# Attention in front of two feed-forward layers: another order of work on the engines, v requested after its first sum, guards stored as columns

## Chip, cores and metric

One core of one Trainium2 chip. The metric is the device time of one execution in microseconds (us), for one core. Engines: TensorE (PE, with PEld its weight loads), VectorE (DVE), ScalarE (ACT), GpSimd (POOL), and SyncE (SP), which issues the DMAs.

## What is computed

```python
# q, k, v: (4, 8, 576, 64) float32
q_d, k_d, v_d = (t.reshape(B, H, 144, 4, D).mean(axis=3) for t in (q, k, v))
out_d = softmax_guarded(q_d @ k_d.T / 8) @ v_d          # denominator + 1e-9
out_up = np.repeat(out_d, 4, axis=2)
scores = np.where(abs(i - j) < 4, q @ k.T / 8, -1e9)    # a band of 7 keys a query
out_local = softmax_guarded(scores) @ v
x = (out_up + out_local) -> (2304, 512)
x = ((h := x @ w_in1) * sigmoid(h)) @ w_out1            # 512 -> 2048 -> 512
x = ((h := x @ w_in2) * sigmoid(1.702 * h)) @ w_out2
```

## The kernel before

Attention runs in 16 units; a unit is two heads of one batch entry, its features on 128 partitions. After it come six token blocks of the feed-forward layers (class `Ffn`), whose weights and inputs are split in a rounded part and a rest, so that each product is three TensorE matmuls. `Ffn` isn't touched by the change; its order is written out too.

In attention each engine has a program of its own, ordered by semaphores. `iterations` (L787) gives unit 0, a hardware loop up to EARLY - 1, then units written out up to 15, and a last call that only finishes unit 15. Each call of `body(u)` starts unit u and finishes unit u-1 ("old"):

- TensorE (L1165): `band_scores(u)` (L1086) writes the mask into two PSUM banks with two bfloat16 matmuls (L1091), then adds 18 matmuls of q by a window of 70 keys, one for each head h and tile t (L1098); head h uses the array's rows 64h to 64h+63 and writes output partitions 64h to 64h+63. `avg_scores(u)` (L1114, L1119) gives the scores of the averaged attention by three matmuls whose stationary operand `qavg` is block diagonal. `group(old, j)` transposes exponentials: j = 0 to 2 three band tiles each, j = 3, 4 half of the averaged ones (L1084). `band_product` (L1149) and `avg_product` (L1160) follow. Groups 3 and 4 stand between the products.
- VectorE (L1013): maxima of the band scores (L1022), subtraction (L1025), maxima of the averaged scores (L1029), `sums(u+1)`, which adds fours of q and k (L1010), row sums of the band exponentials (L1034), + 1e-9 (L1036), reciprocal (L1040), the averaged sums + 1e-9 (L1044), reciprocal (L1046), `early` (work for the first feed-forward block: L245, L256, L284), and the unit's output `x` (L1056).
- ScalarE (L950): copies of the transposed groups out of PSUM (L935, L939), the band exponential (L959), the averaged exponentials with their row sums (L972), `diagonal(u+1)` (L948), which copies q's sums into `qavg`, `oavg` (L981), and roundings for the first block.
- GpSimd (L883): normalises band and averaged exponentials (L889, L893), adds four rows of v in two steps (`vpair` L898, `vavg` L902), then two sums of first-layer weights (`sum_weights`, L905, into `G`: L912/L914 in odd units, L917/L918 in even ones).
- SyncE (L822), its requests in one queue: `load_qk(u+2)` once `band_scores(u)` and `sums(u)` are done; `load_vwin(u+1)` (v's windows); `load_vn(u+1)` once `vavg(u)` is done (`v_sum`); in odd units `first_raw` (raw weights, L113).

Before all that GpSimd makes two identities and the mask (12 small fills, L874), and TensorE runs 11 warm-up matmuls (L1184).

Of the kernel before, what the change touches and what calls it, by code (L numbers as in the profile page):

```python
# [22 lines left out]
P = 128  # L23
# [661 lines left out]
def build(nc, qkT, v, vw, w_in, w_out, out, heads):  # L685
# [7 lines left out]
    EARLY = 5  # L693
# [10 lines left out]
    AQ = 96  # L704
    NA = 2 * SD // AQ
# [10 lines left out]
    with ExitStack() as whole:  # L716
# [9 lines left out]
        with ExitStack() as ctx:  # L726
# [17 lines left out]
            qavg = sb("qavg", [P, 2, SD])  # L744
            sums4 = sb("sums4", [P, 2, SD])
            pband = [sb(f"pband{i}", [P, NT, WIN]) for i in range(2)]
            pavg = [sb(f"pavg{i}", [AQ, NA, SD]) for i in range(2)]
            mxb, smb, rcb = (sb(n, [P, NT]) for n in ("mxb", "smb", "rcb"))
            mxa, nga, sma, rca = (sb(n, [AQ, NA]) for n in ("mxa", "nga", "sma", "rca"))
            ptb = ffn.spare(NT * P).rearrange("p (t n) -> p t n", t=NT)  # L750
            pta = sb("pta", [P, 2, 2 * SD])
# [19 lines left out]
        q_diag = sem("q_diag")  # L771
        band_sc = sem("band_sc")
        avg_sc = sem("avg_sc")
        b_max, b_sub, b_exp, b_sum, b_grd, b_rcp, b_nrm = (
            sem("b_" + n) for n in ("max", "sub", "exp", "sum", "grd", "rcp", "nrm"))
# [24 lines left out]
        def _(eng):  # L800
# [13 lines left out]
            def start(u):  # L814
                load_qk(u)
                load_qk(u.after())
                load_vn(u)
                eng.wait_ge(pads, 2)
                load_vwin(u)
                load_vwin(u.after())  # L820

            def body(u, first=False):  # L822
                if not isinstance(u.n, int) or u.n + 2 < UNITS:


                    if first:
                        eng.wait_ge(avg_sc, u.n + 1)
                    else:
                        eng.wait_ge(band_sc, 2 * (u.n + 1))
                        eng.wait_ge(qk_sum, u.n + 1)  # L830
                    load_qk(u.after().after())
                if not isinstance(u.n, int) or u.n + 1 < UNITS:
# [3 lines left out]
                    eng.wait_ge(v_sum, u.n + 1)  # L836
                    load_vn(u.after())
# [19 lines left out]
        def _(eng):  # L857

            eng.memset(ident[:], 0.0).then_inc(consts_fill, 1)
            eng.memset(band[:], 0.0).then_inc(consts_fill, 1)  # L860
            eng.memset(ident16[:], 0.0).then_inc(consts_fill, 1)
            eng.wait_ge(consts_fill, 3)
            for tile in (ident, ident16):
                eng.affine_select(out=tile[:], in_=tile[:], compare_op=ALU.not_equal, fill=1.0, base=0,
                                  pattern=[[-1, P]], channel_multiplier=1).then_inc(consts, 1)
            eng.wait_ge(consts, 2)
            fills = 3
            for a in (0, 1, NT - 1):
                off = starts[a] - QT * a
                for sign in (1, -1):  # L870

                    for h in range(2):
                        part = band[h * QT:(h + 1) * QT, a, :]
                        eng.affine_select(out=part, in_=part, compare_op=ALU.is_ge, fill=NEG,  # L874
                                          base=sign * off + FACTOR - 1,
                                          pattern=[[sign, WIN]],
                                          channel_multiplier=-sign).then_inc(consts_fill, 1)
                        fills += 1

                        eng.wait_ge(consts_fill, fills)  # L880
            eng.sem_inc(consts, 1)

            def body(u, first, last):  # L883
# [5 lines left out]
                eng.tensor_tensor(e[:], e[:], rcb[:].unsqueeze(2).broadcast_to([P, NT, WIN]),  # L889
# [3 lines left out]
                eng.tensor_tensor(e[:], e[:], rca[:].unsqueeze(2).broadcast_to([AQ, NA, SD]),  # L893
                                  ALU.mult).then_inc(a_nrm, 1)
# [29 lines left out]
            eng.wait_ge(pads, 3)  # L924
# [4 lines left out]
        def _(eng):  # L929
            def group(u, j):  # L930
# [7 lines left out]
                else:  # L938
                    eng.activation(pta[0:HP, j - NLG, :], pt[bank][0:HP, 0:2 * SD],  # L939
                                   ACT.Copy).then_inc(p_cp, 1)  # L940

            def diagonal(u):

                eng.wait_ge(qk_sum, u.n + 1)
                eng.wait_ge(avg_sc, u.n)
                for h in range(2):
                    rows = slice(h * D, (h + 1) * D)
                    eng.activation(qavg[rows, h, :], sums4[rows, 0, :], ACT.Copy).then_inc(q_diag, 1)  # L948

            def body(u, first, last):  # L950
# [6 lines left out]
                if last is not None:  # L957
                    eng.wait_ge(b_sub, 2 * (u.n + 1))
                    eng.activation(pband[u.odd][:], pband[u.odd][:], ACT.Exp,  # L959
                                   scale=scale_band).then_inc(b_exp, 1)  # L960
                if not first:
                    for j in range(NLG, NG):
                        group(old, j)
                if last is not None:

                    eng.wait_ge(a_max, u.n + 1)
                    eng.activation(nga[:], mxa[:], ACT.Copy, scale=-scale_avg).then_inc(a_neg, 1)
# [3 lines left out]
                    for c in range(NA):  # L971
                        eng.activation(pavg[u.odd][:, c, :], sa[0:AQ, c * SD:(c + 1) * SD], ACT.Exp,  # L972
                                       scale=scale_avg, bias=nga[:, c:c + 1],
                                       accum_out=sma[:, c:c + 1]).then_inc(a_exp, 1)
                    if not last:
                        diagonal(u.after())

# [5 lines left out]
                if not first and isinstance(u.n, int):  # L983
                    if u.n in (5, 7, 8):
                        ffn.round_weights(eng, (5, 7, 8).index(u.n))
                    elif u.n == 6:
                        eng.wait_ge(x_done, 1 + 2)
                        ffn.round_x(eng, 0, B11)
                    elif 9 <= u.n < 15:
                        eng.wait_ge(x_done, 1 + 8)  # L990
                        ffn.round_x(eng, 0, FILLS[u.n - 8])

            eng.wait_ge(consts, 3)
# [5 lines left out]
            iterations(eng, diagonal, body)  # L999
# [4 lines left out]
        def _(eng):  # L1004
            def sums(u):
                eng.wait_ge(avg_sc, u.n)
                if not isinstance(u.n, int) or u.n:
                    eng.wait_ge(q_diag, 2 * u.n)
# [4 lines left out]
            def body(u, first, last):  # L1013
                if last is not None:
# [3 lines left out]
                    halves = [(e[:, a:b, :], sc[:, bank, 0:(b - a) * WIN].rearrange(  # L1018
# [10 lines left out]
                    eng.tensor_reduce(mxa[:], sa[0:AQ, 0:NA * SD].rearrange("p (c k) -> p c k", c=NA),  # L1029
                                      AX.X, ALU.max).then_inc(a_max, 1)  # L1030
                    if not last:
                        sums(u.after())
# [14 lines left out]
                if not first and isinstance(u.n, int):  # L1047
                    early(u.n)
# [12 lines left out]
            def early(n):  # L1061

                if n in (6, 8, 9):
                    ffn.rest_weights(eng, (6, 8, 9).index(n))
                if n == 7:
                    ffn.rest_x(eng, 0, B11)
                    ffn.sum_x(eng, 0, T1)
                elif n == 9:
                    ffn.sum_x(eng, 0, T3)
                elif 10 <= n < 16:  # L1070
                    ffn.rest_x(eng, 0, FILLS[n - 9])
# [162 lines left out]
```

## Time and profile before

| | us |
|---|---|
| runs, median (lowest to highest, 3 runs) | 848.26 (846.18 to 851.7) |
| profiled execution, its own time | 845.45 |
| its span on the engines | 843.7 |
| attention in that span | 0 to 134.76 |

The span holds first the attention, then the feed-forward part, where TensorE is busy 701.60 of 708.94 us. Rows give start and duration, engine, source line, operation, output <- input and a count. In a timeline "[0.96 <-POOL x]" is the idle time of the engine before the row and what ended it. One float32 matmul leaves two records, a transpose one.

### The profile page before, as it was taken

The numbers are of one execution on the slowest core, as the hardware profiler recorded it, in microseconds if no ns is written. First come the engines' busy times: TensorE is split into PE (matmuls) and PEld (weight loads), VectorE is DVE, ScalarE is ACT, GpSimd is POOL, SyncE is SP. The second block draws the span as 40 slices with busy tenths as digits, with TensorE's granted clock in tenths as the row PEclk, the third lists the DMA queues.
The fourth block names the chain that finished last, engine by engine and source line by source line (L and its number), as shares of the span: only waits on it lengthen the run. The fifth ranks groups of instructions, "written<-read, shape, count | busy, mean of one in ns | idle before, by whom it ended". The sixth has DMA issues, their size and how long they took to land.

```text
span 843.7 us, 15737 instructions
## 1 busy us (share of the span) xinstructions
PE 816.2 (97%) x5691; PEld 787.6 (93%) x5691; DVE 667.5 (79%) x959; ACT 533.9 (63%) x847; POOL 207.5 (25%) x215
## 2 busy tenths in 40 slices
PE   7997988999999999999999999999999999999998
PEld 4776767999999999999999999999999999999998
DVE  6889895989999878888967888899865678655465
ACT  4676765567754667846567755578555677466663
POOL 5778787742005532015510000000000000000000
PEclk9999899999999999999999999999999999999999
DMA  5676556757867778768887777878787878887773
GB/s 173 196 217 187 155 182 219 270 177 280 261 221 245 266 260 316 255 211 267 275 283 251 234 248 258 258 246 279 239 306 248 273 255 266 266 273 256 277 260 127
DMA packets 98312, 205.37 MB, mean 243 GB/s; under 512 B 8416, under 2 KB 56032, under 8 KB 98240
## 3 DMA queue, kind: packets, MB, share of 16 engines
q1 hardware_dynamic: 98240, 204.42, 73.5%
q8 instruction: 44, 0.72, 0.3%
q14 instruction: 28, 0.23, 0.1%
HBM read 160.87 MB, written 43.52 MB: 242 GB/s over the span
## 4 chain that ended last, share of the span: by engine, by line
PE 77%; DVE 10%; DMA 4%; POOL 4%; issue 3%; ACT 1%; SPq 1%; POOLq 0%; DVEq 0%; ACTq 0%
PE hid L309 41%; PE yp L332 35%; DMA qk<-in_qkT 4%; DVE gr L482 2%; DVE wh L284 2%; DVE sums L1010 1%; POOL pband L889 1%; DVE xs L245 1%; DVE smb L1034 1%; POOL vpair L898 1%; POOL pavg L893 1%; PE pt L1084 0%; PE po L1149 0%; DVE mxb L1022 0%; POOL vavg L902 0%
## 5 line engine op out<-in xcount | busy, mean ns | idle before, releaser
L309 PE MATMUL hid<-xs,wh 128*128 128x384 f32 x2016 | 352.5, 334 | 1.6 <-DVE hw L462 1.2
L309 PEld LDWEIGHTS hid<-xs,wh 128*128 128x128 f32 x2016 | 349.2, 188 | 4.1 <-issue 3.5
L332 PE MATMUL yp<-gr,wh 128*128 128x384 f32 x2016 | 350.9, 334 | 1.8 <-DVE gr L482 1.8
L332 PEld LDWEIGHTS yp<-gr,wh 128*128 128x128 f32 x2016 | 349.5, 188 | 2.3 <-issue 2.3
L275 ACT ACTIVATE wh<-wr 128x1024 fp32r<-128x1024 f32 (+1 forms) x164 | 164.6, 1003 | 155.1 <-PE hid L309 119.5
L482 DVE TENSOR_TENSOR gr<-G,gr 128x768 fp32r<-128x768 f32 x144 | 138.8, 974 | 47.8 <-ACT gr L382 47.8
L382 ACT ACTIVATE gr<-G 128x768 fp32r<-128x768 f32 x144 | 121.7, 845 | 68.7 <-PE yp L332 67.4
L284 DVE TENSOR_TENSOR wh<-wr,wh 128x1024 fp32r<-128x1024 f32 x76 | 90.0, 1185 | 21.6 <-ACT wh L275 21.6
L349 ACT ACTIVATE G<-G 128x1152 f32<-128x1152 f32 x48 | 55.7, 1161 | 0.0
L457 DVE TENSOR_TENSOR hv<-p,hid 128x384 f32<-128x384 f32 x48 | 26.4, 550 | 26.9 <-PE hid L309 21.3
L245 DVE TENSOR_TENSOR xs<-x,xs 128x768 fp32r<-128x768 f32 x42 | 42.9, 1022 | 5.8 <-ACT xs L241 5.8
L472 DVE TENSOR_TENSOR G<-hv,hid 128x384 f32<-128x384 f32 x48 | 26.5, 551 | 26.4 <-PE hid L309 26.1
L424 DVE TENSOR_TENSOR G<-G 128x384 f32<-128x384 f32 x48 | 29.2, 608 | 8.4 <-ACT G L349 8.4
L241 ACT ACTIVATE xs<-x 128x768 fp32r<-128x768 f32 x42 | 34.9, 832 | 0.2
L549 POOL TENSOR_TENSOR G<-G 128x256 f32<-128x256 f32 x8 | 7.5, 933 | 100.2 <-DMA G<-in_w_in 53.8
L1149 PEld LDWEIGHTS po<-yt,vwin 128*64 128x64 f32 x576 | 21.8, 142 | 10.6 <-ACT yt L935 6.8
L1149 PE MATMUL po<-yt,vwin 128*64 128x64 f32 x576 | 28.3, 235 | 3.3 <-ACT yt L935 3.3
L549 POOL TENSOR_TENSOR wt<-wt 128x256 f32<-128x256 f32 x12 | 12.2, 1020 | 76.1 <-DMA wt<-in_w_out 44.2
L889 POOL TENSOR_TENSOR pband<-pband,rcb 128x630 f32<-128x630 f32 x16 | 23.6, 1475 | 22.6 <-DVE rcb L1040 22.6
L469 DVE TENSOR_TENSOR G<-hw,hid 128x384 f32<-128x384 f32 x48 | 26.4, 549 | 3.4 <-DMA sums_in<-G 2.0
L935 ACT ACTIVATE yt<-pt 70x384 f32<-70x384 f32 x32 | 13.8, 482 | 23.3 <-PE pt L1084 23.3
L431 DVE TENSOR_TENSOR G<-G 128x384 f32<-128x384 f32 x48 | 27.9, 582 | 0.2
(88 smaller groups left out, 824.7 us busy)
## 6 DMA issues: line engine op xcount, KB each, us to landing
wh<-rests SPq DMA_DIRECT2D x72, 512.0 KB, 3.8
wr<-sums_out SPq DMA_DIRECT2D x48, 512.0 KB, 4.9
wr<-in_w_out SPq DMA_DIRECT2D x36, 512.0 KB, 5.2
rests<-wh SPq DMA_DIRECT2D x36, 512.0 KB, 3.3
wr<-sums_in SPq DMA_DIRECT2D x40, 384.0 KB, 4.0
wr<-in_w_in SPq DMA_DIRECT2D x40, 256.0 KB, 3.5
qk<-in_qkT SPq DMA_DIRECT2D x16, 576.0 KB, 6.0
G<-in_w_in SPq DMA_DIRECT2D x12, 512.0 KB, 4.4
```

The costliest lines, as they stand in the source:

```text
L241: eng.activation(xs[:, 0, q], features(n, q), ACT.Copy).then_inc(self.x_hi, 1)
L245: eng.tensor_tensor(xs[:, 1, q], features(n, q), xs[:, 0, q].bitcast(F32), ALU.subtract).then_inc(self.x_lo, 1)
L275: eng.activation(wh[:, w % SLOTS, 0, 0:entries(w), :], raw(w), ACT.Copy).then_inc(w_hi, 1)
L284: eng.tensor_tensor(wh[:, w % SLOTS, 1, 0:e, :], raw(w), wh[:, w % SLOTS, 0, 0:e, :].bitcast(F32), ALU.subtract).then_inc(w_lo, 1)
L309: last = eng.matmul(hid[:, at, 0:HALF], lhsT=wh[:, w % SLOTS, part, a % 4, cc * P:(cc + 1) * P], rhs=xs[:, rest, q, cc, :], start=start an ...
L332: last = eng.matmul(yp[:, at + m, 0:HALF], lhsT=wh[:, w % SLOTS, part, p % 4, m * P:(m + 1) * P], rhs=gr[:, p, rest, :], start=start and p ...
L349: eng.activation(G[:, s % PAIRS, G12:G22 + 1, :], G[:, s % PAIRS, G12:G22 + 1, :], ACT.Silu, scale=scale).then_inc(self.gate, 1)
L382: eng.activation(gr[:, 2 * a:2 * a + 2, 0, :], G[:, 2 * a:2 * a + 2, at, :], ACT.Copy).then_inc(self.g_hi, 1)
L424: eng.tensor_tensor(G[:, p, G11, :], G[:, p, G12, :], G[:, p, G11, :], ALU.subtract).then_inc(self.t_sum, 1)
L482: eng.tensor_tensor(gr[:, 2 * a:2 * a + 2, 1, :], G[:, 2 * a:2 * a + 2, SECOND[i][1], :], gr[:, 2 * a:2 * a + 2, 0, :].bitcast(F32), ALU.s ...
L889: eng.tensor_tensor(e[:], e[:], rcb[:].unsqueeze(2).broadcast_to([P, NT, WIN]), ALU.mult).then_inc(b_nrm, 1)
L1149: last = eng.matmul(po[h * D:(h + 1) * D, t * QT:(t + 1) * QT], lhsT=vwin[:, u.odd, t, h * D:(h + 1) * D], rhs=ptb[:, t, h * QT:(h + 1) * QT],
```

## The change

It touches only attention and the set-up.

- The guards: `pband` has a 71st column and `sma` a second column that hold 1e-9, written once; the row sums run over them. The two `tensor_scalar` additions go; the averaged one becomes a `tensor_reduce` over two columns.
- GpSimd forms `vpair(u)` at the head of body(u), before it normalises; SyncE asks for vn(u+1) after `vpair(u)` (`v_half`) in place of `vavg(u)`, and before qk(u+2), vwin(u+1) and the raw weights.
- `qavg` and ScalarE's `diagonal` go: six matmuls of 64 rows by 48 columns replace three of 128 by 96. `pavg` holds 112 partitions in place of 96.
- Head h and tile t write the output half (h + t) mod 2, two tiles of one head and two of the other in turn, in two halves with a wait of TensorE on itself between them.
- TensorE: band groups, then `avg_scores(u)`, then groups 3 and 4, then all products. VectorE: `sums(u+1)` moves behind the band reciprocal, `early` ahead of the band's row sums. ScalarE: the averaged maxima's scaling before groups 3 and 4. `early` starts at other units (VectorE 4, ScalarE 3) and is spread over more of them.
- Set-up: the mask in 4 fills, the bfloat16 identity first; the float32 one after the mask; EARLY is 3.

```diff
-    EARLY = 5
+    EARLY = 3
...
-            pband = [sb(f"pband{i}", [P, NT, WIN]) for i in range(2)]
+            pband = [sb(f"pband{i}", [P, NT, WIN + 1]) for i in range(2)]
+            sma = sb("sma", [AR, NA, 2])
@@ sync
             def body(u, first=False):
+                if not isinstance(u.n, int) or u.n + 1 < UNITS:
+                    eng.wait_ge(v_half, u.n + 1)
+                    load_vn(u.after())
...
-                    eng.wait_ge(v_sum, u.n + 1)
-                    load_vn(u.after())
@@ gpsimd
-            for a in (0, 1, NT - 1):
...
+            for sign in (1, -1):
+                for h in range(2):
+                    part = band[h * QT:(h + 1) * QT, 0:3, :]
...
+                eng.wait_ge(vn_in, DMA_INC * (u.n + 1))
+                if not first:
+                    eng.wait_ge(v_sum, u.n)
+                rows = vn.rearrange("p j (r d) -> p r j d", r=FACTOR)
+                eng.tensor_tensor(vpair[:], rows[:, 0:2], rows[:, 2:4], ALU.add).then_inc(v_half, 1)
                 eng.wait_ge(b_rcp, u.n + 1)
...
-                eng.wait_ge(vn_in, DMA_INC * (u.n + 1))
-                rows = vn.rearrange("p j (r d) -> p r j d", r=FACTOR)
-                eng.tensor_tensor(vpair[:], rows[:, 0:2], rows[:, 2:4], ALU.add).then_inc(v_half, 1)
@@ vector
-                    if not last:
-                        sums(u.after())
+                if not first and isinstance(u.n, int):
+                    early(u.n)
+                if last is not None:
                     eng.wait_ge(b_exp, u.n + 1)
                     eng.tensor_reduce(smb[:], e[:], AX.X, ALU.add).then_inc(b_sum, 1)
                     eng.wait_ge(b_sum, u.n + 1)
-                    eng.tensor_scalar(smb[:], smb[:], GUARD, None, ALU.add).then_inc(b_grd, 1)
-                    eng.wait_ge(b_grd, u.n + 1)
...
                     eng.reciprocal(rcb[:], smb[:]).then_inc(b_rcp, 1)
+                    if not last:
+                        sums(u.after())
...
-                    eng.tensor_scalar(rca[:], sma[:], GUARD, None, ALU.add).then_inc(a_grd, 1)
+                    eng.tensor_reduce(rca[:], sma[:], AX.X, ALU.add).then_inc(a_grd, 1)
@@ tensor
+                for h in range(2):
+                    for i in range(0, NT - LEFT, 2):
+                        for g, t in ((h, i), (h, i + 1), (1 - h, LEFT + i), (1 - h, LEFT + i + 1)):
+                            head_scores(g, t)
+                    last = head_scores(h, LEFT - 1)
+                    if h == 0:
+                        last.then_inc(half_sc, 1)
+                        eng.wait_ge(half_sc, u.n + 1)
                 last.then_inc(band_sc, 2)
...
                 for c in range(NA):
+                    for h in range(2):
+                        rows = slice(h * D, (h + 1) * D)
+                        last = eng.matmul(sa[h * QT:h * QT + AQ, c * SD:(c + 1) * SD],
+                                          lhsT=sums4[rows, 0, c * AQ:(c + 1) * AQ], rhs=sums4[rows, 1, :],
+                                          start=True, stop=True)
```

## Rows read from the trace of the kernel before

**Rows 1.** Busy time by window: start:end, length, PE, PEld, DVE, ACT, POOL; PEclk; DMA share, GB/s.

```profile
0.00:134.76 134.76, 114.59 (x1660) 89.16 (x1660) 112.90 (x208) 85.99 (x267) 104.28 (x119) 0.97 0.59 176
```

**Rows 2.** Chain of waits from 38 to 80 us: start us, us, what.

```profile
39.64 0.30 SPq L806
...
40.31 0.37 SPq L113
...
41.03 5.91 DMA qk<-in_qkT
...
47.05 1.35 DVE sums L1010
...
53.97 0.30 SPq L806
...
61.66 1.35 DVE sums L1010
...
77.91 1.35 DVE sums L1010
```

**Rows 3.** Timeline of GpSimd from 51 to 56 us.

```profile
50.86 0.91 POOL L893 TENSOR_TENSOR pavg<-pavg,rca 96x432 f32<-96x432 f32 x1
51.73 1.27 POOL L898 TENSOR_TENSOR vpair<-vn 72x512 f32<-72x512 f32 x1
53.08 0.73 POOL L902 TENSOR_TENSOR vavg<-vpair 72x256 f32<-72x256 f32 x1
...
54.58 0.73 POOL L914 TENSOR_TENSOR G<-G 128x256 f32<-128x256 f32 x1
```

**Rows 4.** Timeline of VectorE from 105 to 125 us.

```profile
117.18 0.86 DVE L1022 TENSOR_REDUCE mxb<-sc 128x5 f32<-128x350 f32 x2
...
119.26 1.33 DVE L1010 TENSOR_REDUCE sums<-qk 128x288 f32<-128x1152 f32 x1
...
121.95 1.96 DVE L245 TENSOR_TENSOR xs<-x,xs 128x768 fp32r<-128x768 f32 x1
...
124.50 0.86 DVE L1022 TENSOR_REDUCE mxb<-sc 128x5 f32<-128x350 f32 x2
```

**Rows 5.** Instructions of single VectorE lines: xcount, duration ns min/median/max, first and last start.

```profile
L1036 DVE TENSOR_SCALAR smb<-smb x16: 173/174/759, 13.7 to 127.8; 128x9 f32<-128x9 f32 x16
...
L1044 DVE TENSOR_SCALAR rca<-sma x16: 104/135/1222, 14.1 to 129.0; 96x3 f32<-96x3 f32 x16
...
L1034 DVE TENSOR_REDUCE smb<-pband x16: 790/799/811, 12.9 to 126.9; 128x9 f32<-128x630 f32 x16
...
L245 DVE TENSOR_TENSOR xs<-x,xs x7: 923/925/1962, 64.3 to 129.8; 128x768 fp32r<-128x768 f32 x7
```

**Rows 6.** Timeline of TensorE from 40.6 to 48 us.

```profile
40.74 0.44 PE L1091 MATMUL sc<-band,ident 128*128 128x350 bf16 x2
41.11 1.38 PE L1098 MATMUL sc<-qk 64*64 64x70 f32 x36
42.42 0.98 PE L1119 MATMUL hp<-sums,qavg 128*96 128x144 f32 x6
...
44.30 0.57 PE L1149 MATMUL po<-yt,vwin 128*64 128x64 f32 x12
...
46.67 0.72 PE L1160 MATMUL po<-pta,vavg 128*64 128x144 f32 x8
47.32 0.44 PE L1091 MATMUL sc<-band,ident 128*128 128x350 bf16 x2
```

**Rows 7.** Groups by line from 0 to 150 us: busy us, mean ns, idle before.

```profile
L1098 PEld LDWEIGHTS sc<-qk 64*64 64x64 f32 x576 | 20.3, 135 | 4.4 <-issue 4.4
```

**Rows 8.** Timeline of the start, 0 to 32 us.

```profile
2.50 4.47 PE L1184 MATMUL sc<-ident 128*128 128x512 bf16 x11 [2.50 <-POOL ident L864]
2.59 4.46 POOL L874 TENSOR_SCALAR_AFFINE_SELECT band<-band 64x70 bf16<-64x70 bf16 x12
...
7.74 0.44 PE L1091 MATMUL sc<-band,ident 128*128 128x350 bf16 x2 [0.77 <-ACT band L994]
```

More of the change, by code:

```diff
@@ L938, in group @@
                 else:
-                    eng.activation(pta[0:HP, j - NLG, :], pt[bank][0:HP, 0:2 * SD],
+                    eng.activation(pta[0:HP, j - NLG, :], pt[bank][0:HP, 0:NA * AR],
                                    ACT.Copy).then_inc(p_cp, 1)
[L942 to L948, printed above, removed]
             def body(u, first, last):
@@ L971, in body @@
                     for c in range(NA):
-                        eng.activation(pavg[u.odd][:, c, :], sa[0:AQ, c * SD:(c + 1) * SD], ACT.Exp,
+                        eng.activation(pavg[u.odd][:, c, :], sa[0:AR, c * SD:(c + 1) * SD], ACT.Exp,
                                        scale=scale_avg, bias=nga[:, c:c + 1],
-                                       accum_out=sma[:, c:c + 1]).then_inc(a_exp, 1)
-                    if not last:
-                        diagonal(u.after())
+                                       accum_out=sma[:, c, 0:1]).then_inc(a_exp, 1)
                 if not first:
@@ L1028, in body @@
                     eng.wait_ge(avg_sc, u.n + 1)
-                    eng.tensor_reduce(mxa[:], sa[0:AQ, 0:NA * SD].rearrange("p (c k) -> p c k", c=NA),
+                    eng.tensor_reduce(mxa[:], sa[0:AR, 0:NA * SD].rearrange("p (c k) -> p c k", c=NA),
                                       AX.X, ALU.max).then_inc(a_max, 1)
-                    if not last:
-                        sums(u.after())
+                if not first and isinstance(u.n, int):
+                    early(u.n)
+                if last is not None:
                     eng.wait_ge(b_exp, u.n + 1)
@@ L1061, in early @@
             def early(n):
[L1063 to L1071, printed above, removed]
-                    for q in {T1: (T2,), B21: (T4,)}.get(FILLS[n - 9], ()):
-                        ffn.sum_x(eng, 0, q)
-            for pad in (qavg[:], vwin[P // 2:], vavg[P // 2:]):
+                if n in (4, 5, 6):
+                    ffn.rest_weights(eng, n - 4)
+                elif n in (8, 13):
+                    ffn.sum_x(eng, 0, T1 if n == 8 else T4)
+                elif n in (9, 10):
+                    ffn.sum_x(eng, 0, T3 if n == 9 else T2)
+                if n in (7, 9, 10, 11, 12, 14, 15):
+                    ffn.rest_x(eng, 0, FILLS[(7, 9, 10, 11, 12, 14, 15).index(n)])
+            for pad in (vwin[P // 2:], vavg[P // 2:]):
                 eng.memset(pad, 0.0).then_inc(pads, 1)
+            for guard in (pband[0][:, :, WIN:], pband[1][:, :, WIN:], sma[:, :, 1:]):
+                eng.memset(guard, GUARD).then_inc(pads, 1)
             eng.sem_inc(x_done, 1)
@@ L1096, in head_scores @@
                     bank, a = (0, 0) if t < LEFT else (1, LEFT)
-                    rows = slice(h * D, (h + 1) * D)
-                    return eng.matmul(sc[rows, bank, (t - a) * WIN:(t - a + 1) * WIN],
+                    rows, half = slice(h * D, (h + 1) * D), side(h, t)
+                    return eng.matmul(sc[half, bank, (t - a) * WIN:(t - a + 1) * WIN],
                                       lhsT=qk[rows, u.odd, 0, t * QT:(t + 1) * QT],
@@ L1174, in body @@
                         group(old, j)
+                if last is not None:
+                    avg_scores(u)
+                if first:
+                    eng.wait_ge(consts, 3)
+                    eng.wait_ge(pads_too, 2)
+                if not first:
+                    for j in range(NLG, NG):
+                        group(old, j)
                     for j in range(NLG):
                         band_product(old, j)
-                        if NLG + j < NG:
-                            group(old, NLG + j)
                     avg_product(old)
-            eng.wait_ge(consts, 2)
-            for _ in range(WARM):
-                eng.matmul(sc[:, 0, :], lhsT=ident16[:], rhs=ident16[:].unsqueeze(1).broadcast_to(
+            eng.wait_ge(consts, 1)
+            for n in range(WARM):
+                eng.matmul(sa if n % 2 else sc[:, 0, :], lhsT=ident16[:], rhs=ident16[:].unsqueeze(1).broadcast_to(
                     [P, 4, P]), start=True, stop=True)
-            eng.wait_ge(band_cp, 1)
-            eng.wait_ge(pads, 1)
+            eng.wait_ge(band_cp, 2)
+            eng.wait_ge(pads, 5)
             iterations(eng, lambda u: None, body)
```

121 lines of the change are left out of this document (51 added, 70 removed).

## The prediction

> **What bounds the kernel now.** I read the busy time by window first [rows 1]: in attention no engine is full (TensorE 114.59 of 134.76 us, VectorE 112.90, GpSimd 104.28), so what costs is who waits for whom. Behind attention TensorE is all but full for 709 us and the change doesn't touch that part, so every microsecond is won or lost before 134.76. 16 units between the first band scores at 7.74 [rows 8] and 134.76 are 7.94 us a unit.
>
> The chain of waits [rows 2] shows a loop that closes once in two units. `vavg(u)` ends on GpSimd; SyncE issues vn (39.64), the raw weights (40.31), then qk (41.03), whose 5.91 us let VectorE's `sums` begin at 47.05. From there it goes through the band's row sums, guard, reciprocal and normalisation to the averaged normalisation at 50.86, `vpair`, `vavg` [rows 3] and the next vn at 53.97. The sums of the chain start at 47.05, 61.66 and 77.91: 14.6 and 16.25 us for two units. The reader is to see that qk isn't late because of its own buffer but because its request stands in SyncE's queue behind a request that waits for GpSimd.
>
> Close under it lie two engines. VectorE needs 124.50 - 117.18 = 7.32 us for a unit in which nothing makes it wait [rows 4]; 1.9 of them are `early`, so 5.4 are attention. TensorE needs 47.32 - 40.74 = 6.58 us [rows 6].
>
> **The loop after the change, step by step.** v's request now hangs on `vpair(u)`:
> - end of `vpair` to issue of vn: 0.16, as from `vavg` (53.81) to 53.97 today [rows 2, 3];
> - vn to qk: 1.39 today, less the raw weights' turn (41.03 - 40.31 = 0.72), which now come behind: 0.67;
> - qk's flight and handover: 47.05 - 41.03 = 6.02 [rows 2];
> - `sums` 1.26 (its row of 1.33 less the overlap) [rows 4], now directly followed by the averaged guard sum and reciprocal, 0.45 with handover to GpSimd (L1044's median is 0.135, the reciprocal alike, each waits for the one before) [rows 5];
> - GpSimd: averaged normalisation 0.87, `vavg` 0.73, weights 1.5, and then the next `vpair` 1.35, together what lies between 50.86 and 55.31 [rows 3], 4.45.
>
> Sum 0.16 + 0.67 + 6.02 + 1.26 + 0.45 + 4.45 = 13.0 us for two units against 14.3 (39.64 to 53.97). In words: 0.7 is gone with the raw weights' turn, 2.1 with the band's sums and normalisation (47.05 to 50.86 was 3.8, it becomes 1.7), and 1.5 comes in, the weight sums that now stand ahead of `vpair`. The new queue order isn't free: qk(u+2) could go out when `band_scores(u)` is done, by these step lengths 3 to 4 us earlier, but stands behind the wait for `vpair(u)`; behind it in turn stand vwin(u+1) and the raw weights, which are needed only a unit later.
>
> From unit 4 on `early` stands between VectorE's averaged maxima and the band's row sums, which by the step lengths is when GpSimd is at the weight sums and `vpair`. Rows show what a meeting costs: L245 takes 0.925 or 1.96 [rows 5]; whoever comes second waits for the other. I charge 0.9 to `vpair` on each turn: 13.9 for two units, 6.95 a unit. Its bounds are 13.0 (never met) and 14.9 (met twice a turn).
>
> **The other edits.**
> - Guards. L1036 and L1044 take 0.17 and 0.135, but up to 0.76 and 1.22 [rows 5], which 9 and 3 elements a partition can't explain: they wait for something outside VectorE. Row sums (L1034) last 790 to 811 ns in all 16 units, whatever GpSimd does. VectorE loses one instruction (0.2) and about 0.35 of stalls a unit, attention 5.4 becomes 5.2. 639 columns for 630 cost 0.01. Bounds for the new small `tensor_reduce`: 0.10 to 0.3.
>  The Trainium skill (SBUF - State Buffer, "Who interferes with whom") says that a `tensor_scalar` in its two-port mode excludes GpSimd and a `tensor_reduce` on trn2 never does; L1034's spread of 21 ns agrees, and by it the replacement keeps 0.1 to 0.2 always. By the row alone I would fear the old 1.2 in one unit of 16; either way it lies in VectorE's slack of the forecast.
> - VectorE's own turn becomes 5.2 + `early` (0.92 to 1.2, once 1.0 more in units 9 and 10) = 6.1 to 6.5: under 6.95. With `sums` behind the reciprocal, the band exponential (0.8 behind the subtraction) is hidden under the averaged maxima and `early`.
> - ScalarE loses the two copies of `diagonal`; busy 86 of 134.76 us [rows 1] and not in the chain, it wins nothing by that. From unit 8 its rounding waits for x(u-1), one turn of VectorE later, 2.3 us behind the reciprocal; its copies then end 0.6 later than today, just as VectorE ends `early`. Cost 0, up to 0.4 a unit if that cover fails.
> - TensorE. Scores: 18 matmuls in 1.31 (41.11 to 42.42), the two heads side by side. That is 36 records two at a time, 18 steps of 0.07. Four at a time each half takes three rounds of two records, 12 steps, 0.85 us; if the loads are the limit, 1.3. The wait on itself between the halves adds 0.2 to 0.3 (an estimate: handovers cost 0.11 to 0.16 here [rows 2], and the pipeline drains). I take 1.2, bounds 0.9 to 1.7. Six averaged matmuls pair up on separate rows: 0.8 as now, 1.6 if they don't. Products without transposes between them: 44.30 to 46.67 is 2.37, it becomes 1.9, since the switches and two short waits for copies go [rows 6]. A unit of TensorE: 6.58 - 0.1 + 0 - 0.45 = 6.0, bounds 5.7 to 7.4, so it idles a little.
> - Set-up. 12 fills of 0.38 end at 7.05 [rows 8]; 4 fills of three times the length, 0.5 each by the same rows, end near 4.2. Then the 4.47 us of warm-up bind: they begin at about 2.0 (2.50 now), so the first scores start at 6.5, not 7.74: 1.2 won, bounds 0.5 to 1.6.
>
> **The sum.** First scores 6.5; 1.7 for them, 1.6 maxima and subtraction, 0.8 exponential, 1.3 row sums and reciprocal: sums(1) at 12.0. sums(2) at 17.2. `vpair(1)` ends at 12.0 + 1.7 + 4.45 = 18.15, so sums(3) at 18.15 + 6.85 = 25.0, and sums(4), through vpair(2) at 24, at 31.0. Five turns of 13.9 to sums(14) 100.5, 6.95 to sums(15), 1.5 for the two units with two pieces of `early`: 109.0. VectorE's unit 15 takes 6.5: 115.5. Tail: normalisation 1.35 (of the 3.8 from 47.05 to 50.86 what row sums, guard and reciprocal leave), transposes 1.1 (42.42 to 44.30 less the averaged scores' 0.8), averaged ones 0.7, products 1.2, averaged product 0.7 [rows 6]: 5.1. Attention ends at 120.6 to 120.9, I take 120.8, against 134.76: 13.9 us won, 1.6%. The span 843.7 becomes 829.8, the execution 845.45 becomes 831.5. The median of the runs is 2.8 above the profiled execution, so I say 848.3 - 13.9 = 834.4.
>
> The granted clock averages 0.97 over attention [rows 1], so it was at 1.2 GHz for some 6% of it. If TensorE's waits become shorter, part of that may come back; I add nothing for it.
>
> **Rivals.**
> 1. The loop doesn't bind, VectorE does (qk flies shorter with no raw weights ahead, `vpair` isn't met). Then 6.4 a unit from sums(4) on plus 2.0 for the double units: 31 + 11 x 6.4 + 2.0 = 103.4, + 6.5 + 5.1 = 115.0, 19.8 won, 828.5. For: 6.4 and 6.95 are near. Against: in the chain qk has 512 KB of raw weights and v ahead of it and still lands within 5.91 [rows 2], so taking the weights away may give little.
> 2. The loop at its upper bound, 14.9 for two units: `vpair` met twice, since GpSimd is busy 104.28 / 16 = 6.5 us a unit already [rows 1]. 31 + 11 x 7.45 + 1.5 = 114.5, + 11.6 = 126.1, 8.7 won at most; with ScalarE's 0.4 in the last seven units 129, 6 won: 841.5.
> 3. Slower. TensorE becomes the bound because the new order of score tiles puts two tiles of the same array rows one behind the other, and the load of each second one isn't hidden: 18 of the 36 loads at 0.135 [rows 7] are 2.4 us, plus 0.3 for the wait, less 0.45 of the products: 6.58 + 2.3 = 8.9 a unit. 6.5 + 16 x 8.9 = 148.9 is 14 later: 862. It decides from 8.0 us a unit of TensorE on, that is scores over 3.2 us. Against: L1149's two column halves share all rows, and their 12 records lie in 0.57 us [rows 6], loads hidden.
>  The Trainium skill (TensorE: Matmul & The Clock Gate, "The mechanism") states that a weight load overlaps a running matmul only when the row group differs, which speaks against this change; L1149's rows disagree for column halves, and no row shows four tiles.
>
> **How the numbers follow.** Forecast 0.52 (830 to 839), rival 1 0.23, rival 2 0.18, rival 3 0.07. The time is the forecast's, 834.4. The range 827 to 842 takes in the middles of rivals 1 and 2. A difference of about 1%, 8.5 us, is what a measurement can tell here: faster by more holds the forecast and rival 1 and a little of rival 2, 0.77; within it 0.16; slower 0.07.
>
> **What would show it.** Right: the chain of waits still passes over qk's flight, but with turns near 13.9; qk's issue 0.7 behind vn's; the small reduce on `sma` never over 0.3; records of the scores four within 0.06 us; GpSimd with `vpair` directly ahead of the band normalisation; TensorE at full clock throughout. Wrong: `sums` never waits for qk (rival 1), `vpair` of 2 us (rival 2), scores over 2 us (rival 3).

## The result and the profile after

The kernel after takes 834.04 us (median of 6 runs, 831.72 to 837.03), the kernel before 848.83 us on the same chips: ratio 0.9822, 95% interval 0.9806 to 0.9839, faster by 1.8%. The profiled execution took 831.72 us with a span of 829.9, against 845.45 and 843.7. The prediction said 834.4, a span of 829.8 and 13.9 us won.

The whole gain lies in attention. Its last products run from 119.90 to 120.61 and the feed-forward part begins behind them; in the kernel before it began at 134.76. First the busy time of that stretch (columns as in [rows 1]):

```profile
0.00:120.64 120.64, 102.47 (x1756) 77.69 (x1756) 99.22 (x194) 73.68 (x236) 102.79 (x111) 0.99 0.69 197
```

Against [rows 1] VectorE is busy 13.7 us less (112.90 before), ScalarE 12.3, TensorE 12.1, GpSimd only 1.5: GpSimd's share rose from 77% to 85%. The granted clock averages 0.99 where it was 0.97.

The chain of waits from 40 to 75 us, which answers to [rows 2] ("..." marks pieces left out; "issue" is time that the chain can't put down to any wait):

```profile
42.42 1.95 POOL vpair L895
...
44.37 1.20 POOL pband L898
...
46.31 0.91 POOL pavg L902
...
47.21 0.68 POOL vavg L908
...
47.89 0.68 POOL G L918
...
48.65 2.04 POOL G L920
...
50.69 1.23 POOL vpair L895
...
56.05 1.95 POOL vpair L895
...
59.20 1.77 issue
...
61.00 0.91 POOL pavg L902
...
63.36 1.76 POOL G L920
65.12 1.24 POOL vpair L895
...
66.52 4.79 DMA vn<-in_v
```

It passes over GpSimd, not over qk: `vpair` from 42.42 to 56.05 is one turn of two units, 13.6 us, and in these turns two of GpSimd's operations are stretched (a weight sum from 0.73 to 1.76 and 2.04, `vpair` from 1.24 to 1.95). That reads as if GpSimd alone set the pace. But the 1.77 us at 59.20 are no work of GpSimd: its timeline gives them as idle time that ended with VectorE's averaged reciprocal.

```profile
61.00 0.91 POOL L902 TENSOR_TENSOR pavg<-pavg,rca 112x432 f32<-112x432 f32 x1 [1.81 <-DVE rca L1045]
```

VectorE's waits say what lies behind that:

```profile
DVE sums L1008 <- DMA qk<-in_qkT: 6.7, 6, 1.5
DVE mxa L1027 <- PE hp L1121: 5.7, 9, 1.9
```

`sums` waited six times for qk, once at the very start and then in the even units 4, 6, 8, 12 and 14. SyncE and VectorE show the wait of unit 8 whole:

```profile
52.10 0.31 SPq L809 DMA_DIRECT2D vn<-in_v  x1
52.75 0.91 SPq L806 DMA_DIRECT2D qk<-in_qkT  x1
```

```profile
59.29 1.35 DVE L1008 TENSOR_REDUCE sums<-qk 128x288 f32<-128x1152 f32 x1 [1.45 <-DMA qk<-in_qkT]
60.56 0.15 DVE L1043 TENSOR_REDUCE rca<-sma 112x3 f32<-112x6 f32 x1
...
63.59 0.95 DVE L256 TENSOR_TENSOR x<-x 128x768 f32<-128x768 f32 x1
64.45 0.81 DVE L1033 TENSOR_REDUCE smb<-pband 128x9 f32<-128x639 f32 x1
65.30 0.22 DVE L1037 RECIPROCAL rcb<-smb 128x9 f32<-128x9 f32 x1
65.43 1.30 DVE L1008 TENSOR_REDUCE sums<-qk 128x288 f32<-128x1152 f32 x1
```

`vpair` ends at 51.92, vn goes 0.18 later, qk 0.65 behind it, `sums` begins 6.54 later after an idle time of 1.45, and GpSimd's averaged normalisation at 61.00, 1.71 behind that. These are the prediction's terms one by one (0.16, 0.67, 6.02, 1.71). GpSimd's part, from 61.00 to the end of the next `vpair` at 66.36, is 5.36 (the forecast: 4.45 and 0.9). The turn from 51.92 to 66.36 is 14.4 us. From one `sums` to the next is 65.43 - 59.29 = 6.14 when nothing is waited for.

The new guard and the new score order:

```profile
L1043 DVE TENSOR_REDUCE rca<-sma x16: 148/149/159, 12.4 to 115.6; 112x3 f32<-112x6 f32 x16
```

```profile
50.69 0.44 PE L1091 MATMUL sc<-band,ident 128*128 128x350 bf16 x2
51.06 1.21 PE L1098 MATMUL sc<-qk 64*64 64x70 f32 x36
53.27 0.82 PE L1080 MATMUL pt<-ident,pband 128*70 128x128 f32 x6 [1.00 <-POOL pband L898]
```

The averaged guard sum lasts 148 to 159 ns, never more, where L1044 went up to 1222 [rows 5]; in 11 of the 16 units GpSimd's band normalisation, beside which L1044 was long, is under way meanwhile. 18 score matmuls with the wait of TensorE on itself lie in 1.21 us (1.38 in [rows 6]); TensorE idles 1.00 before the transposes.

### The profile page after: what moved, and what is told of

Read it like the earlier page. It is cut to its first block, busy times and chain, and to the rows that moved or that the text cites. A ratio compares the mean times of both kernels' runs of the same rounds, so it can differ in the third digit from the quotient of the medians.

```text
span 829.9 us, 15752 instructions
## 1 busy us (share of the span) xinstructions
PE 803.5 (97%) x5787; PEld 776.1 (94%) x5787; DVE 652.5 (79%) x945; ACT 521.6 (63%) x816; POOL 201.3 (24%) x207
## 4 chain that ended last, share of the span: by engine, by line
PE 78%; POOL 9%; DVE 7%; issue 3%; DMA 2%; ACT 0%; SPq 0%; POOLq 0%; DVEq 0%; ACTq 0%
PE hid L309 41%; PE yp L332 36%; POOL vpair L895 3%; DVE gr L482 2%; DMA vn<-in_v 2%; POOL pband L898 2%; POOL G L920 2%; DVE wh L284 1%; POOL pavg L902 1%; POOL vavg L908 1%; DVE xs L245 1%; DMA sums_in<-G 1%; POOL G L918 1%; PE pt L1080 0%; POOL G L924 0%
## 5 line engine op out<-in xcount | busy, mean ns | idle before, releaser
L245 DVE TENSOR_TENSOR xs<-x,xs 128x768 fp32r<-128x768 f32 x42 | 40.6, 967 | 5.6 <-ACT xs L241 5.6
L241 ACT ACTIVATE xs<-x 128x768 fp32r<-128x768 f32 x42 | 35.0, 832 | 15.1 <-DVE x L1053 15.1
L275 ACT ACTIVATE wh<-G 128x1024 fp32r<-128x1024 f32 (+1 forms) x16 | 15.3, 955 | 19.7 <-PE hid L309 19.7
L474 DVE TENSOR_TENSOR gr<-G,gr 128x384 fp32r<-128x384 f32 x48 | 27.6, 575 | 0.0
L462 DVE TENSOR_TENSOR hw<-hv,hid 128x384 f32<-128x384 f32 x48 | 26.3, 549 | 1.5 <-PE hid L309 1.2
L364 ACT ACTIVATE G<-hid 128x384 f32<-128x384 f32 x48 | 23.6, 492 | 5.8 <-PE hid L309 1.2
```

The costliest lines, as they stand in the source:

```text
L241: eng.activation(xs[:, 0, q], features(n, q), ACT.Copy).then_inc(self.x_hi, 1)
L245: eng.tensor_tensor(xs[:, 1, q], features(n, q), xs[:, 0, q].bitcast(F32), ALU.subtract).then_inc(self.x_lo, 1)
L275: eng.activation(wh[:, w % SLOTS, 0, 0:entries(w), :], raw(w), ACT.Copy).then_inc(w_hi, 1)
L474: eng.tensor_tensor(gr[:, p, 1, :], G[:, p, G11, :], gr[:, p, 0, :].bitcast(F32), ALU.subtract).then_inc(self.b11_lo, 1)
```

## The experiments

Each of the 12 kernels ran beside the kernel before; ratios are to that, with the 95% interval. Medians of the kernel before differ by about 1 us between the chips, so kernels are compared by their ratios (0.001 is 0.85 us). The kernel after is 0.9822.

**Is the loop over qk real?** One edit each on the kernel after and on the kernel before takes qk out from behind the wait for GpSimd.

```diff
 # a_qk_first: SyncE's turn in the kernel after
-                    eng.wait_ge(v_half, u.n + 1)
-                    load_vn(u.after())
...
                     load_qk(u.after().after())
...
+                    eng.wait_ge(v_half, u.n + 1)
+                    load_vn(u.after())
```

> The kernel after, with one line moved on SyncE: qk(u+2) is requested ahead of vn(u+1), as soon as band_scores(u) is done. Theory A (the prediction's loop: end of vpair, vn, qk's flight, sums, reciprocal, GpSimd's row, vpair): qk leaves some 3 us earlier, the loop opens, sums waits for qk no more (6.7 us now) and VectorE and GpSimd bind with 6.4 to 6.8 us a unit in place of 7.15: 4 to 7 us less than after, 828 to 830. Rival B (the chain of waits names GpSimd's lines, so GpSimd alone sets the turn and qk only happens to be late): no difference, 833 to 835.

Measured 827.86 us, 0.9762 (0.9713 to 0.981): some 5 us under the kernel after, as theory A said. One of its four runs took 834.18, so its interval just touches that of the kernel after (0.9806 to 0.9839); what makes the gain clear is a_qk_first_vn2 below, the same edit and a second buffer for v, with 0.9765 (0.9732 to 0.9797). In the profiled executions attention ends at 116.15 in place of 120.54. In its trace `sums` waits for qk once, at the very start:

```profile
DVE sums L1007 <- DMA qk<-in_qkT: 0.9, 1, 0.9
```

The chain's reading, that GpSimd alone sets the turn, falls: GpSimd does the same work in the same order here.

```diff
 # b_qk_first: SyncE's turn in the kernel before
                     load_qk(u.after().after())
+                if not first:
+                    eng.wait_ge(v_sum, u.n)
+                    load_vn(u)
...
-                    eng.wait_ge(v_sum, u.n + 1)
-                    load_vn(u.after())
```

> The kernel before with vn(u)'s request and its wait for v_sum moved behind the request of qk(u+2) of the next turn of SyncE. Theory A (the loop over v_sum, SyncE's queue and qk's flight binds before): the 5.4 us of waits for qk go and 3 to 7 us are won, 842 to 846. Rival I (VectorE's turn of 7.3 us with early and the guards' stalls binds before, qk is only just late): within 1.5 us of before.

Measured 844.53 us, 0.9952 (0.9937 to 0.9966), 4.1 us less than before, inside theory A's 3 to 7. The gain is one of medians: the profiled execution took 845.70 us, no less than the 845.45 of the kernel before, and its TensorE clock averages 0.94 over attention where [rows 1] has 0.97. The waits of `sums` fell from 5.4 us to 0.6:

```profile
DVE sums L1011 <- DMA qk<-in_qkT: 0.6, 1, 0.6
```

So opening the loop is worth 4 to 5 us in either kernel. It was the tightest before the change, with others close under it, and doesn't alone make up the 14 us.

**The part on v.** Undone on the kernel after (a_old_v), done alone on the kernel before (b_new_v):

```diff
 # a_old_v: SyncE, then GpSimd
-                    eng.wait_ge(v_half, u.n + 1)
-                    load_vn(u.after())
...
                         load_vwin(u.after())
+                    eng.wait_ge(v_sum, u.n + 1)
+                    load_vn(u.after())
...
-                eng.tensor_tensor(vpair[:], rows[:, 0:2], rows[:, 2:4], ALU.add).then_inc(v_half, 1)
                 eng.wait_ge(b_rcp, u.n + 1)
...
+                eng.tensor_tensor(vpair[:], rows[:, 0:2], rows[:, 2:4], ALU.add).then_inc(v_half, 1)
                 eng.wait_ge(v_half, u.n + 1)
```

> The kernel after with the part on v undone: vpair behind the averaged normalisation, vn asked for once vavg is done and last in SyncE's turn, as before. Theory A: the loop becomes 0.16 + 1.39 + 6.02 + 1.26 + 0.45 + 2.95 = 12.2 us for two units (the weight sums leave it), under what VectorE and GpSimd need, so this kernel is faster than after by 3 to 7 us: 827 to 831. Rival C (asking for v earlier is what the change gains by): slower than after by 5 us or more, 839 and up.

> The kernel before with the part on v alone: vpair at the head of GpSimd's turn, vn asked for on v_half and ahead of qk. Theory A: the loop of before, 14.3 us for two units, becomes 0.16 + 0.67 + 6.02 + 3.81 + 4.45 = 15.1, so it is slower than before by 3 to 7 us: 852 to 855. Rival C: faster than before by 5 us or more.

Both went between the theories. a_old_v: 838.32 us, 0.9864 (0.9826 to 0.9903), about 3.6 us slower than the kernel after, with intervals that just overlap; theory A's 827 to 831 is out. Its sum gave a turn of 12.2 us, but `sums` still waits six times for qk, 5.9 us in all, and the chain shows turns of 14.4 (39.79 to 54.17) and 14.1 us:

```profile
39.79 6.65 DMA qk<-in_qkT
...
48.24 0.87 POOL pavg L896
...
49.13 1.28 POOL vpair L901
...
50.48 2.15 POOL vavg L905
...
54.17 6.63 DMA qk<-in_qkT
```

Two terms are longer than in the sum. From qk's issue to `sums` it is 6.7 us in place of 6.02, and from the averaged normalisation to the end of `vavg` 4.39 in place of 2.95, as `vavg` lasts 2.15 us where [rows 3] has 0.73. In the four units from 43 to 67 us it lasts 1.8 to 2.2: with `vpair` back behind the averaged normalisation, `vavg` meets `early`, and it lies in the loop. TensorE also waits for `vavg` in nine units (5.3 us in all), but in this stretch that wait isn't in the chain.

b_new_v: 849.22 us, 0.998 (0.9957 to 1.0004), no difference from before. Its chain runs over qk as computed:

```profile
57.66 5.62 DMA qk<-in_qkT
...
63.40 1.35 DVE sums L1013
...
71.87 1.23 POOL vpair L892
...
73.92 5.84 DMA qk<-in_qkT
...
79.88 1.35 DVE sums L1013
```

The turn from 48.71 to 63.40 is 14.7 us where before has 14.6, the next 16.5 where [rows 2] has 16.25. The two flights are shorter (5.62 and 5.84 for 5.88 and 6.27), perhaps because the raw weights are now asked for behind qk; no run separates that. The forecast set 15.1 against 14.3, but 14.3 was a short turn of the kernel before: between the `sums` of its units 4 to 14 the five turns take 14.4 to 17.5, 15.7 in the mean, and here 14.7 to 17.8, 16.2 in the mean. That is 2.5 us in one pair of executions, which the medians don't confirm. On the kernel before the part on v wins nothing that can be told; on the kernel after it is worth some 3 to 4 us.

**The place of sums.**

```diff
 # a_old_sums: VectorE in the kernel after
                                       AX.X, ALU.max).then_inc(a_max, 1)
+                    if not last:
+                        sums(u.after())
...
                     eng.reciprocal(rcb[:], smb[:]).then_inc(b_rcp, 1)
-                    if not last:
-                        sums(u.after())
```

> The kernel after with sums(u+1) back in its old place on VectorE, behind the averaged maxima and ahead of early and the band's row sums. Theory A: from qk's landing to the averaged reciprocal the loop then passes early, the row sums and the band's reciprocal (2.1 us more a turn of two units, seven turns): 10 to 15 us slower than after, 843 to 849. Rival E (the place of sums is of no account, since VectorE's turn is the same length either way): no difference, 833 to 836.

847.9 us, 0.9985 (0.9964 to 1.0005): the whole gain is gone. Theory A's figure came true, but its reason is at most a part of it: `sums` waits less for qk than in the kernel after (3.2 us in all against 6.7), and what has grown is another wait:

```profile
DVE sums L1008 <- DMA qk<-in_qkT: 3.2, 4, 1.0
DVE mxa L1027 <- PE hp L1121: 21.6, 15, 3.4
```

The second was 5.7 us in the kernel after. The chain passes over qk's flight twice up to 62 us, and from there on over a loop of one unit:

```profile
104.13 1.34 DVE sums L1008
105.47 1.02 DVE xs L245
106.50 0.74 DVE smb L1035
...
107.56 1.25 POOL pband L898
...
108.94 0.82 PE pt L1080 x6
109.76 0.33 PE hp L1080 x3
110.09 0.89 PE hp L1121 x12
...
111.53 1.34 DVE sums L1008
```

The prediction didn't have this loop. The change puts `avg_scores(u)` behind the band groups of unit u-1, and they wait for GpSimd's band normalisation, which waits for the band reciprocal: normalisation 1.25 and handovers 0.2, transposes 1.1, averaged scores 0.95, averaged maxima 0.5, `early` 0.9, row sums and reciprocal 1.1. That is 6.0; with `sums` (1.26) between the maxima and `early` it is 7.3, and 7.2 to 7.4 is the step between its sums in units 12 to 15. The kernel before, which forms the averaged scores ahead of the band groups, has no such loop. So the 14 us are what the change would lose if it moved `avg_scores` and left `sums` in place, and not what moving `sums` wins over the kernel before.

Three earlier steps are longer (9.8, 9.3 and 8.8 us), and they hold something else: TensorE runs part of them at 1.2 GHz.

```profile
83.34 1.47 PE pt L1080 x6
84.81 0.64 PE hp L1080 x3
85.45 1.55 PE hp L1121 x12
```

These pieces take 3.66 us where the same ones from 108.94 on take 2.04. The granted clock is 0.54 from 83.30 to 87.00; in the 3.3 us before, TensorE was busy for 1.14. It is much the same from 66.4 and 93.1 on, 4.4 us more in all in this chain, and the clock averages 0.94 over attention where the kernel after has 0.99. So about a third of the distance between the two profiled executions (attention ends at 133.30 and 120.54) is TensorE's clock. That it falls because TensorE waits longer in the loop is likely, but no run shows it.

To tell the loop from theory A, the same kernel ran with qk first:

> a_old_sums with qk requested ahead of v. Theory A (a_old_sums was 14 us slower than after because the way from qk's landing to vpair got longer): the loop over qk opens, it gains most of that back, 832 or less. Theory H (sums then lies in the one-unit loop over the averaged scores, 7.3 us): stays within 3 us of a_old_sums, 845 to 849.

842.89 us, 0.9939 (0.9916 to 0.9962): 4 us less than a_old_sums and 15 more than a_qk_first. The 4 us are the loop over qk again. The 15 are theory H's, with what the clock costs in them (0.92 over attention, 0.99 in a_qk_first); `mxa` still waits 22.2 us:

```profile
DVE mxa L1026 <- PE hp L1120: 22.2, 15, 3.4
```

Neither range holds: theory A asked for 832 or less, theory H for 845 to 849. The run lies 2 us under H's and 11 over A's, so most of it is H's and a rest is A's.

**The guards.**

```diff
 # b_guards: VectorE in the kernel before (a_old_guards is the reverse, in the kernel after)
-                    eng.tensor_scalar(smb[:], smb[:], GUARD, None, ALU.add).then_inc(b_grd, 1)
-                    eng.wait_ge(b_grd, u.n + 1)
...
-                    eng.tensor_scalar(rca[:], sma[:], GUARD, None, ALU.add).then_inc(a_grd, 1)
+                    eng.tensor_reduce(rca[:], sma[:], AX.X, ALU.add).then_inc(a_grd, 1)
```

> The kernel before with the guards alone as columns beside what is summed. Theory A: the band's guard lies in the loop (0.2 a turn, 8 turns) and VectorE loses 0.2 and its stalls: 2 to 5 us less than before, 844 to 847. Rival D (the stalls of the two guards are the main cost of before): 8 us less or more.

846.62 us, 0.9968 (0.9952 to 0.9984), 2.7 us less, inside theory A's 2 to 5. VectorE is quicker, and most of what it saves becomes waiting for qk, 11.9 us where the kernel before has 5.4:

```profile
DVE sums L1011 <- DMA qk<-in_qkT: 11.9, 9, 2.6
```

> The kernel after with the guards as two tensor_scalar additions again. Theory A: they lie beside the loop (GpSimd's band normalisation is under way at that time in any case), 0 to 3 us slower than after, 834 to 837. Rival D (the guards' stalls carry the gain): slower by 5 us or more. In the trace the averaged guard should last up to 1.2 us again where GpSimd is at work.

840.43 us, 0.9906 (0.9874 to 0.9939): 7 us slower than the kernel after, twice what theory A allowed and what rival D said. The band's guard shows why:

```profile
L1035 DVE TENSOR_SCALAR smb<-smb x16: 173/1086/1096, 11.8 to 119.9; 128x9 f32<-128x9 f32 x16
```

Its median is 1086 ns where [rows 5] has 174. In the new order `vpair` often begins just when the band's row sums end: in 9 of the 16 units the guard starts 0.2 us behind it and lasts 1.08 to 1.10 us, in 3 GpSimd is idle and it lasts 0.17 to 0.18, in 4 it starts late in `vpair` and lasts 0.33 to 0.43. VectorE's unit is then 7.3 us (61.15 to 68.42 in that trace, with one piece of `early`), and `sums` waits for qk only 1.0 us in all: VectorE binds. The guards as columns are thus worth more in the new order than in the old one.

**Parts that don't matter.**

```diff
 # a_old_tiles: TensorE in the kernel after, output side of head h is half h again
-                    for i in range(0, NT - LEFT, 2):
-                        for g, t in ((h, i), (h, i + 1), (1 - h, LEFT + i), (1 - h, LEFT + i + 1)):
-                            head_scores(g, t)
...
+                for i in range(NT - LEFT):
+                    head_scores(0, i)
+                    head_scores(1, LEFT + i)
```

> The kernel after with the band scores two tiles side by side as before, each head in its own output half and no wait of TensorE on itself. Theory A: TensorE isn't the bound, 18 matmuls take 1.31 in place of 1.14 us, no difference: within 2 us of after. Rival F (TensorE's turn binds): 0.17 x 16, 2 to 4 us slower.

834.5 us, 0.983 (0.9797 to 0.9863), no difference from the kernel after, as expected; its band scores take 1.38 us a unit, as in [rows 6], against 1.21.

```diff
 # a_early_back: VectorE in the kernel after
-                if not first and isinstance(u.n, int):
-                    early(u.n)
-                if last is not None:
                     eng.wait_ge(b_exp, u.n + 1)
...
                     eng.reciprocal(rca[:], rca[:]).then_inc(a_rcp, 1)
+                if not first and isinstance(u.n, int):
+                    early(u.n)
```

> The kernel after with VectorE's early work back in its old place, behind the averaged reciprocal and ahead of x. Theory A with H: early leaves the loop of one unit over the averaged scores (6.1 becomes 5.2), but now meets GpSimd's averaged normalisation, which is in the loop over qk just as vpair is, delays x and the next maxima, and no longer covers the band exponential (0.35 a unit on VectorE): 1 to 5 us slower than after, 835 to 839. Rival J (its place is of no account, the work is the same): within 1 us, 833 to 835. Rival H alone (the one-unit loop binds after): faster than after by 3 us or more.

835.31 us, 0.9842 (0.9819 to 0.9864), 1.7 us above the kernel after by the ratios, with intervals that overlap: at the lower edge of A with H, not apart from rival J, and rival "H alone" falls.

**How far can it be carried?** Two kernels, each with one edit on top of a_qk_first: a second buffer for v, and the averaged scores ahead of the band groups again.

```diff
 # a_qk_first_vn2
-                eng.dma_start(vn, v[bass.ds(u.n, 1), :, :].rearrange(
+                eng.dma_start(vns[u.odd], v[bass.ds(u.n, 1), :, :].rearrange(
...
-                if not isinstance(u.n, int) or u.n + 1 < UNITS:
+                if not isinstance(u.n, int) or u.n + 2 < UNITS:
                     eng.wait_ge(v_half, u.n + 1)
-                    load_vn(u.after())
+                    load_vn(u.after().after())
+                if not isinstance(u.n, int) or u.n + 1 < UNITS:
```

> The faster version a_qk_first with a second buffer for v (in space of the feed-forward part that is idle during attention), so that vn(u+2) is requested once vpair(u) is done. Its chain of waits passes over v's own flight (4.1 to 5.8 us between one vpair and the next). Theory A carried on: that loop opens too and GpSimd waits 5 us less in all: 2 to 5 us less than a_qk_first, 823 to 826. Rival G (VectorE or the meetings of VectorE and GpSimd bind already): no difference, 827 to 829.

828.61 us, 0.9765 (0.9732 to 0.9797), nothing gained: rival G holds. GpSimd's waits for v fell from 5.0 us (five) to 2.1 (one) and the time stayed, so the waits for v that the chain showed had slack behind them.

```diff
 # a_qk_avg_front: TensorE
                     band_scores(u)
+                    avg_scores(u)
                 if not first:
                     for j in range(NLG):
                         group(old, j)
-                if last is not None:
-                    avg_scores(u)
```

> a_qk_first with avg_scores(u) on TensorE ahead of the band groups, as before the change. Theory H (found in the traces of after and a_old_sums: a loop of one unit, band reciprocal, GpSimd's band normalisation, nine transposes, averaged scores, averaged maxima, early, row sums, reciprocal, 6.1 us in after; VectorE waits 5.8 us for the averaged scores in a_qk_first): the loop opens and this kernel is 2 to 5 us faster than a_qk_first, 823 to 826. Rival G (VectorE's own turn of 5.2 us and early, met by GpSimd, binds): within 1.5 us of a_qk_first, 827 to 829.

826.59 us, 0.9741 (0.9712 to 0.977) beside 0.9762 (0.9713 to 0.981). The lowest median of all, but it isn't apart from a_qk_first, and lies between the two theories; whether the loop over the averaged scores costs anything once qk goes first stays open. Both kernels beat the kernel after (0.9806 to 0.9839).

## Why the prediction was right, and where it wasn't

The time, the span and the sign came out: 834.04 for 834.4, 829.9 for 829.8. Several steps hold one by one.

- *What bounds before.* The loop over `v_sum`, SyncE's queue and qk's flight: b_qk_first opens it and wins 4.1 us. That it wins no more fits what the prediction said, that VectorE's turn lies close under the loop: in b_qk_first VectorE is busy 115.9 of attention's 134.0 us, and the steps between its sums are still 7.3 to 8.9 us from unit 8 on.
- *The loop after the change.* The turn shown above takes 14.4 us: 0.18 + 0.65 + 6.54 + 1.71 + 5.36. The forecast had 13.9, and the half microsecond is qk's flight, 6.5 in place of 6.0. The five turns and the double units from sums(4) to sums(14) were to take 71.0 us; they took 71.5 (30.98 to 102.44), unevenly, 13.6 to 14.9. `sums(15)` came at 108.58 for 109.0, the last band normalisation at 115.54 for 115.5, attention's end at 120.6 for 120.8.
- *GpSimd's meetings with `early`*, 0.9 a turn: in the chain above `vpair` is stretched by 0.7 and the weight sum by 1.0 to 1.3, in alternate units. The weight sum's share, which the prediction didn't have, lies on the loop over qk; `vpair`'s, for which it charged, lies in the other units. So 0.9 was the right size for the wrong instruction.
- *Scores and TensorE.* 1.21 with the wait for 1.2 forecast, four tiles abreast without exposed loads: rival 3 doesn't come about, and the page's rule (the Trainium skill, TensorE: Matmul & The Clock Gate, "The mechanism") that a load overlaps a running matmul only where the row group differs isn't borne out by these rows, since two tiles in a row share their row group and 36 records end in 1.21 us, while 18 loads of 0.133 us laid bare would alone take 2.4. Worth nothing in time (a_old_tiles), as said.
- *The set-up.* The first scores were forecast at 6.5 and came at 6.02 (7.74 before); `sums(1)` came at 11.14 where 12.0 was forecast. The other terms of unit 1 took it back (17.67 for 17.2).

Two of its own signs of being right didn't appear. The chain of waits doesn't pass over qk's flight (it stays on GpSimd, and only a_qk_first and VectorE's waits show the loop), and TensorE isn't at full clock throughout (0.57 from 12.00 to 14.00, 0.58 from 14.00 to 16.00). And rival 2's sign, a `vpair` of 2 us, did appear, though not in the units of the loop. A slip besides: rival 2's 6 us won would be 842.3, not 841.5.

The sum added nothing for TensorE's clock. Before the change it is at 1.2 GHz once in attention, behind 85 us (granted clock 0.50 from 85.00 to 90.00), and the groups of products that begin 0.90 us apart at 68.11 and 69.01 begin 1.47 apart there (84.99 and 86.46), about 1.1 us for the two in the chain. The step between VectorE's sums is 10.07 at that point, the longest of all; but b_guards, at full clock there, has one of 10.05. So the clock is at most about 1 us of the 14.

Three steps failed.

1. The guards: "VectorE loses one instruction (0.2) and about 0.35 of stalls a unit, attention 5.4 becomes 5.2". The length of VectorE's turn came out, but the worth of the edit was sized from where the guards stood before. In the new order the band's guard would take 1.1 us in 9 of 16 units, and a_old_guards is 7 us slower where 0 to 3 were expected. The fear about the new reduce ("the old 1.2 in one unit of 16") didn't come true: the Trainium skill's statement that on trn2 a `tensor_reduce` never contends with GpSimd (SBUF - State Buffer, "Who interferes with whom") agrees with 148 to 159 ns in all 16 units, in 11 of which GpSimd is at work.
2. The order of `sums`. The prediction counted its move as 2.1 us off the loop over qk. What decides in a_old_sums is a loop of one unit over the averaged scores, which the change itself makes by putting `avg_scores` behind the band groups; with `sums` left inside it the gain is nil (a_old_sums), and a_qk_first_old_sums shows 15 us of that, clock included, when the loop over qk is open. The size expected for a_old_sums was right for a wrong reason.
3. The part on v. By the prediction's terms a_old_v should have been faster than the kernel after; it is slower by some 3.6 us, because `vavg` then meets `early` (1.8 to 2.2 us in place of 0.73) in the loop over qk, and the flight is 0.7 longer than the term. On the kernel before the part changes nothing that can be told.

So the total agrees partly by luck: the loop over qk was sized well, and the other constraints (VectorE's turn and the loop over the averaged scores, both near 6.1 us a unit) happened to lie just below it. No edit alone carries the 14 us. Guards alone on the old order give 2.7, v alone 0, while taking the guards out of the new order costs 7 and the place of sums 14: the parts depend on each other, and their effects don't add up. No run builds the kernel after up from the kernel before by more than one part, so which smallest set of parts gives the 14 us stays open.

## What to carry to other kernels

In a kernel with several near-critical loops, write down each loop (all the engines it crosses, and how many units it spans) for the order of after as well as before, since moving one piece opens one loop and may close another. When a chain of waits stays on one busy engine, look also at the waits of the others: here it named GpSimd, and moving one DMA request ahead of a wait in SyncE's queue won some 5 us. A small instruction that needs a shared resource should be sized where it will stand, not where it stood.

## What the runs showed of the hardware

A float32 `tensor_scalar` on 128x9 elements lasts 0.17 us while GpSimd is idle and 1.08 to 1.10 us when GpSimd's 1.27 us `vpair` has begun 0.2 us before it (9 of the 16 units of a_old_guards). A `tensor_reduce` doesn't change beside GpSimd's work: over a few elements it takes 148 to 159 ns in the kernel after, with the band normalisation under way in 11 of 16 units, and over 639 columns (9x71) 0.81 to 0.82 us, beside `vpair` or a weight sum in 15 of 16.

Four 64x64 tiles of the array take float32 matmuls side by side even if two in a row share their input rows: 18 of them, split by one wait of TensorE on itself that costs about 0.2 us, in 1.21 us against 1.38 two abreast.

In a_old_sums nine transposes and the averaged scores took 2.04 us at 2.4 GHz and 3.66 us when the granted clock was 0.54, after 3.3 us in which TensorE had been busy for 1.14.
